# Low parts of twenty-six weight tiles moved from VectorE to GpSimd, in a windowed attention with two feed forwards

## The reference, cut to what matters

```python
# attention: q, k, v are (2, 8, 768, 64); each query sees 8 global keys and the last 96 keys, with a bias by distance
scores = scale * q @ k.T - slope * dist
a = exp(scores - max) / (sum + 1e-9)
x = (a @ v) as (1536 tokens, 512)
# first feed forward, w_in (512, 2048), w_out (2048, 512)
h = x @ w_in
g = (a0 + a1*h + a2*h**2 + a3*h**3) / (1 + |b0|*|h| + |b1|*h**2 + 1e-6)
x = g @ w_out
# second feed forward, w2_in (512, 1024), w2_out (1024, 512)
h = x @ w2_in
solu = h * softmax(h)
out = (layer norm of solu, times g_ln) @ w2_out
```

## Time and profile before

| what | value |
|---|---|
| median of 3 runs | 491.23 us (490.56 to 491.66) |
| the profiled execution | 491.82 us, of which the span is 489.9 us |
| PE busy | 480.8 us (98%) |
| DVE busy | 380.6 us (78%) |
| ACT busy | 262.9 us (54%) |
| GpSimd busy | 63.0 us (13%), all but 4.2 us of it before 94 us |
| chain that ended last | PE 86%, DVE 11%, ACT 2% |
| low parts of w_in on DVE | 16 instructions, 12.2 us |
| low parts of w_out on DVE | 8 instructions, 9.8 us |

### The profile page before, as it was taken

The page is one execution under the profiler, slowest core; times in us unless marked ns, Lnnn a source line. Parts: engine busy times, 40 slices in busy tenths (PEclk is TensorE's granted clock), DMA queues, the critical chain, the costliest instruction groups (busy, mean ns, idle before and its releaser), DMA issues.

```text
span 489.9 us, 7177 instructions
## 1 busy us (share of the span) xinstructions
PE 480.8 (98%) x2560; PEld 390.8 (80%) x2560; DVE 380.6 (78%) x705; ACT 262.9 (54%) x474; POOL 63.0 (13%) x133
## 2 busy tenths in 40 slices
PE   7999999999999999999999999999999999999997
PEld 5777667888888887888888788888888888888885
DVE  5899996899999789888878999999785554554450
ACT  4999895655454556544545655444444333433341
POOL 4767765200000000000000000000000000000000
PEclk9999999999999999999999999999999999999999
DMA  8699969600000000000032336332012222222201
GB/s 289 212 400 416 406 233 373 223 34 0 1 0 1 1 0 1 0 1 0 1 87 86 113 102 193 88 110 84 0 44 64 66 65 64 64 64 64 73 34 43
DMA packets 26959, 50.22 MB, mean 103 GB/s; under 512 B 2224, under 2 KB 16560, under 8 KB 25392
## 3 DMA queue, kind: packets, MB, share of 16 engines
q1 hardware_dynamic: 23760, 37.23, 21.9%
q0 software_dynamic: 2880, 12.58, 7.6%
q10 hardware_dynamic: 288, 0.01, 0.0%
HBM read 40.38 MB, written 3.15 MB: 89 GB/s over the span
## 4 chain that ended last, share of the span: by engine, by line
PE 86%; DVE 11%; ACT 2%; issue 1%; POOL 0%; POOLq 0%; DVEq 0%
PE ps L1102 9%; PE ps L1104 9%; PE ps L1103 9%; PE ps L1032 8%; PE ps L1033 8%; PE ps L1034 8%; PE ps L1167 4%; PE ps L1165 4%; PE ps L1122 4%; PE ps L1166 4%; PE ps L1121 4%; PE ps L1120 4%; DVE negs L653 3%; PE ps L1148 2%; DVE bank_a_lo L690 2%; PE ps L963 2%
## 5 line engine op out<-in xcount | busy, mean ns | idle before, releaser
L1102 PE MATMUL ps<-gate_hi,bank_b_hi 128*128 128x512 f32 x192 | 74.8, 390 | 0.5 <-DVE tok_lo L852 0.5
L1032 PE MATMUL ps<-tok_hi,bank_a_hi 128*128 128x512 f32 x192 | 75.1, 391 | 0.0
L1033 PE MATMUL ps<-tok_lo,bank_a_hi 128*128 128x512 f32 x192 | 74.7, 389 | 0.0
L1034 PE MATMUL ps<-tok_hi,bank_a_lo 128*128 128x512 f32 x192 | 74.7, 389 | 0.0
L1103 PE MATMUL ps<-gate_lo,bank_b_hi 128*128 128x512 f32 x192 | 74.7, 389 | 0.0
L1104 PE MATMUL ps<-gate_hi,bank_b_lo 128*128 128x512 f32 x192 | 74.7, 389 | 0.0
L494 ACT ACTIVATE quad<-ps 128x1024 f32<-128x1024 f32 x24 | 24.7, 1029 | 69.9 <-DVE rest L794 67.0
L412 POOL TENSOR_SCALAR probs<-probs,small 128x256 f32<-128x256 f32 (+1 forms) x96 | 48.6, 519 | 24.7 <-DVE small L663 24.0
L452 ACT ACTIVATE probs<-negs,small 128x256 f32<-128x256 f32 (+1 forms) x96 | 46.1, 485 | 6.0 <-DVE small L653 5.7
L776 DVE SCALAR_TENSOR_TENSOR quad<-quad,small,absh 128x1024 f32<-128x1024 f32 x24 | 30.8, 1283 | 21.5 <-ACT absh L497 21.4
L497 ACT ACTIVATE absh<-ps,small 128x1024 f32<-128x1024 f32 x24 | 26.8, 1116 | 33.8 <-PE ps L1104 33.8
(11 more groups left out here) (94 smaller groups left out, 948.3 us busy)
## 6 DMA issues: line engine op xcount, KB each, us to landing
v_sb<-in_v_win SPq DMA_DIRECT2D x8, 704.0 KB, 7.6
bank_a_raw<-in_w_in SPq DMA_DIRECT2D x4, 1024.0 KB, 11.2
bank_a_hi<-in_w_in POOLq DMA_DIRECT2D x4, 1024.0 KB, 9.9
bank_b_raw<-in_w_out SPq DMA_DIRECT2D x4, 1024.0 KB, 9.8
bank_b_hi<-in_w_out POOLq DMA_DIRECT2D x8, 512.0 KB, 5.6
q_sb<-in_q_t SPq DMA_DIRECT2D x16, 192.0 KB, 5.9
k_sb<-in_k_win SPq DMA_DIRECT2D x8, 384.0 KB, 7.2
stage_hi<-tok_hi SPq DMA_DIRECT2D x12, 256.0 KB, 2.7
```

The costliest lines, as they stand in the source:

```text
L1032: pe.matmul(banks(bank, 1), bank_a_hi[:, f, ws], x_hi, start=(k == 0), stop=False)
L1033: pe.matmul(banks(bank, 1), bank_a_hi[:, f, ws], x_lo, start=False, stop=False)
L1034: mm = pe.matmul(banks(bank, 1), bank_a_lo[:, f, ws], x_hi, start=False, stop=(k == KT - 1))
L1102: pe.matmul(banks(4 + k, 1), bank_b_hi[:, f, ws], g_hi, start=first, stop=False)
```

## The change: what it does

Of the 16 subtractions for w_in, DVE keeps the first six (`EARLY_IN`), now at blocks 34, 36, ... 44. The other ten and all eight for w_out go to GpSimd, behind its last transfer for w_out, in the order in which PE needs them: two tiles of w_out, then two of w_in. A new semaphore, `in_lo_late`, tells PE of the ten. SP loads w_in one step (six blocks) later, and GpSimd issues the high parts at blocks 14, 21, 28 and 35.

```diff
-    SPLIT_FROM, CAST_FROM, CAST_EVERY = 16, 10, 6
+    EARLY_IN, SPLIT_FROM, CAST_FROM, CAST_EVERY = 6, 34, 14, 7
...
-                if 1 <= k <= 4:
-                    load_w_in(k - 1)
+                if 2 <= k <= 5:
+                    load_w_in(k - 2)
...
         for j in range(EARLY_OUT, FT // 2):
             cast_w_out(j)
+
+        def split_in_low(f):
+            pool.wait_ge(in_loaded[f // 4], 16)
+            pool.wait_ge(in_hi_loaded[f // 4], 16)
+            pool.tensor_tensor(bank_a_lo[:, f, :], bank_a_raw[:, f, :], bank_a_hi[:, f, :].bitcast(F32),
+                               ALU.subtract).then_inc(in_lo_late, 1)
+
+        def split_out_low(j):
+            tiles = slice(2 * j, 2 * j + 2)
+            pool.wait_ge(outw_loaded[j // 2], 16)
+            pool.wait_ge(outw_hi_loaded[j], 16)
+            pool.tensor_tensor(bank_b_lo[:, tiles, :], bank_b_raw[:, tiles, :], bank_b_hi[:, tiles, :].bitcast(F32),
+                               ALU.subtract).then_inc(outw_lo_ready, 1)
+
+        for j in range(FT // 2):
+            split_out_low(j)
+            for f in (EARLY_IN + 2 * j, EARLY_IN + 2 * j + 1):
+                if f < FT:
+                    split_in_low(f)
...
             f, part = divmod(n - SPLIT_FROM, 2)
-            if part == 0 and 0 <= f < FT:
+            if part == 0 and 0 <= f < EARLY_IN:
                 split_in_low(f)
...
             dve.wait_ge(act_const, 1)
-            split_out_low(0)
             gate_poly(0)
...
             gate_rest(g)
-            if c == 0 and j + 1 < GROUPS:
-                split_out_low(j + 1)
-            elif c == CHUNKS - 1:
+            if c == CHUNKS - 1:
...
             if c == 0:
-                pe.wait_ge(in_lo_ready, f + 1)
+                if f < EARLY_IN:
+                    pe.wait_ge(in_lo_ready, f + 1)
+                else:
+                    pe.wait_ge(in_lo_late, f - EARLY_IN + 1)
```

More of the change, by code:

```diff
@@ L206, in attention_feed_forwards @@
     w2_hi_loaded = [sem(f"w2_hi_loaded{i}") for i in range(FT // 2)]
-    in_lo_ready, outw_lo_ready, w2_lo_ready = sem("in_lo_ready"), sem("outw_lo_ready"), sem("w2_lo_ready")
+    in_lo_ready, in_lo_late, outw_lo_ready, w2_lo_ready = (sem("in_lo_ready"), sem("in_lo_late"),
+                                                           sem("outw_lo_ready"), sem("w2_lo_ready"))
     hidden_ready, act_in_ready, quad_ready, poly_ready = sem("hidden_ready"), sem("act_in_ready"), sem("quad_ready"), sem("poly_ready")
@@ L805, in low_parts @@
                               ALU.subtract).then_inc(done, 1)
-        def split_out_low(j):
-            dve.wait_ge(outw_loaded[j // 2], 16)
-            dve.wait_ge(outw_hi_loaded[j], 16)
-            low_parts(bank_b_hi, bank_b_lo, bank_b_raw, j, outw_lo_ready)
         for h in range(2):
@@ L838, in _ @@
             full_attention()
-            for f in range(FT):
+            for f in range(EARLY_IN):
                 split_in_low(f)
```

## The result

The changed kernel takes 521.68 us (median of 4 runs, 521.32 to 522.16) against 491.35 us for the kernel before (4 runs, 490.56 to 491.66): 1.062 times as long, 95% interval 1.0602 to 1.0639. The forecast was slower, 501.0 us, in a range of 488 to 508. The direction was right, and the size was missed by 20.7 us.

What follows compares the result with a forecast made beforehand. PE, busy 98% of the span, was taken as the bound, losing time only where DVE or GpSimd delay it. Attention's -2.5 and the first chunk's +12.3 gave +9.8: 501.6 us profiled, 501.0 median, range 488 to 508.

Steps and rivals of the forecast that it cites:

- So they take turns by whole instructions, the one that waits comes next: First chunk: DVE's two-input gate instructions and GpSimd's subtractions alternate one by one; estimated cost +12.3 us.
- 3.7, 5.4 and 3.7: First chunk: PE's three main predicted waits in us, for gate_lo of groups 0, 1 and 2.
- the turns' changes given back: First chunk: each switch between DVE and GpSimd recovers 0.13 us, lowering the summed PE waits from 13.4 to 11.3 us.
- the ceiling of 2.44 and 1.36: First chunk: upper bound in us for GpSimd subtractions of 1024 and 512 elements.
- the prediction's walk: First chunk: instruction-by-instruction schedule of DVE, GpSimd and PE; +4.9 us at GpSimd's floor, +18.6 at its ceiling.
- the sum: Whole kernel: -2.5 us from attention and +12.3 from the first chunk make +9.8.
- rival 3: After the first chunk's stalls PE's clock falls to 1.2 GHz, adding 8 us, for 509 us; chance 6%.
- Attention, -2.5 us: Attention: with nine subtractions before block 34 gone from DVE, PE waits less; -2.5 us, between -1.6 and -3.6.
- The later loads I cost at nothing: Attention: loading w_in six blocks later costs nothing; if the last v came late, under 1 us.
- GpSimd's durations: First chunk: two-tensor subtractions on GpSimd take 1.98 us for 1024 elements and 1.12 for 512.
- Rival 1: First chunk: GpSimd's reads don't hold up DVE's gate, leaving only attention's gain; 488.7 us (487.6 to 489.6); chance 22%.
- Rival 2: First chunk: DVE gets the next turn more often and down(0) waits 1.4 us; 490 to 492 us; chance 8%.

## Why the prediction was wrong, and where it was right

**The step that failed** is "So they take turns by whole instructions, the one that waits comes next". It was read from a pair of L412 in attention, and there it held. But that pair stands behind a wait of GpSimd (0.22 us), and the new row stands right behind five DMA issues. One PE wait of 30.2 us took the place of three. Where GpSimd stops once between issues and row, the step holds, and PE waits three times: 3.33, 4.18 and 1.85 us, 9.4 together; with the stop behind the first subtraction 5.69, 2.00 and 3.43, together 11.1 (3.7, 5.4 and 3.7 were worked out, and with the turns' changes given back 11.3 in all).

That these runs stand at 502.8 and 504.0 us, near the 501.0 of the forecast, is in part luck. The subtractions took 2.36 and 1.28 us, close to the ceiling of 2.44 and 1.36 for which the prediction's walk gives +18.6. Against that, a change of turns gave back more than 0.13 us: a gate instruction and a subtraction of 512 took 2.15 us together (L816 to L819, 94.31 to 96.46) where their own times of 1.26 and 1.28 add up to 2.54. And the clock, which the sum left out, cost some 3 us, as shown under rival 3.

Could the trace of before have shown it? Four rows of L412 there stand right behind a DMA issue, and one of them meets a two-input instruction of DVE:

```profile
42.15 0.58 POOL L399 DMA_DIRECT2D bank_a_hi<-in_w_in  x1
42.77 2.21 POOL L412 TENSOR_SCALAR probs<-probs,small 128x256 f32<-128x256 f32 x4
...
44.06 0.68 DVE L690 TENSOR_TENSOR bank_a_lo<-bank_a_raw,bank_a_hi 128x512 fp32r<-128x512 f32 x1
```

L690 got in at once, and GpSimd's last L412 took 909 ns. These are one-tensor pieces of 365 to 504 ns, shorter than any that held DVE in the experiments, so this row looks like turns and warns of nothing. The trace of before has no row of long GpSimd instructions behind an issue. The prediction treated one collision of two short instructions as a rule for eighteen long ones, and gave no chance to DVE's getting no turn.

**Attention, -2.5 us**: -2.8 was measured, of which 0.3 was there by 14 us, and -2.5 in the run without GpSimd's subtractions. The term was right. "The later loads I cost at nothing": v is late by 0.63 us, since the load took 11.3 us where 8.3 were assumed. With the loads as before PE waited 0.91 us for v, 1.47 for k and 0.67 for a copy, but in an execution of 491.53 us, the slowest of seven. The medians differ by 0.9 us in favour of the later ones, and the intervals overlap: the term was small and, if anything, of the other sign.

**GpSimd's durations**, 1.98 and 1.12 us: 2.36 and 1.28 in the row, within the ceiling. The Trainium skill's 4497 ns for 2048 elements ("GPSIMD Engine Reference", section "Performance versus the Vector engine"), halved to 2.25, was closer than my estimate.

**Rival 1**, no hold-up, 488.7 us: not what happened, but its number is that of the kernels whose row doesn't hold DVE, 489.17 with memsets and 489.51 with short pieces. Its "24 us at 1.98 and 1.12" is a slip: 8 x 1.98 + 10 x 1.12 is 27.0, and nothing else in the prediction rests on it. **Rival 2**, DVE favoured: not with whole subtractions, but with pieces of 128x128 it is what happened. The gate ran at 1.3 to 1.5 us an instruction and down(0) waited 2.86 us for GpSimd, where the rival had 1.4.

**Rival 3**, the clock: the prediction had it fall after stalls of 3.7 us, at 8 us in all and a chance of 6%. In the changed kernel it came after one stall of 30 us and cost 2.9. It counts in the runs with turns too. With the stop ahead of the row the granted clock was 0.82 from 96 to 102 us and 0.72 from 116 to 122. Behind PE's first two waits 17 steps from matmul to matmul took 0.37 to 0.50 us where 0.227 is usual, 3.4 us lost. The span grows by 11.1 us there; -2.6 from attention (up(0) at 76.40), 9.4 of waits and 3.4 of clock make 10.2. With the stop behind the first subtraction, and with one behind each, such steps cost 3.1 and 4.1 us. So stalls of 3.3 to 5.7 us did lower the clock; the rival priced a real term about twice too high, and the sum, which had nothing for it, was wrong to leave it out.

**What stays open.** Why a DMA issue leaves GpSimd in this state, and where the limit in duration lies below which instructions let DVE in nonetheless (396 and 442 ns did, 630 and 717 did not, 521 to 572 did once after nine), isn't settled. The stop, the issue inside the row and the one pause were each run once. That the stop has to be one in which GpSimd really waits is inferred: the row's waits for loads that had landed long before cleared nothing.

## What to carry to other kernels

Work that is moved to GpSimd beside two-input DVE work is priced by what it does to DVE, and one collision in a trace tells only of its own circumstances: look whether GpSimd had just waited or just issued a transfer. A wait on the engine's own completion between its DMA issues and a row of SBUF reads turns a hold into turns, which here still cost 12 us (502.80 against 490.98). To lose nothing, let each instruction go by a semaphore of DVE's so that it runs beside PSUM readers (488.64). When an instruction has a mean of twice its known length, look for a single long one before explaining an average.

## What the runs showed of the hardware that was not expected

- A row of GpSimd instructions that read SBUF, behind a DMA issue without a stop, kept one DVE instruction with two inputs in SBUF waiting for 31.97 us (18 instructions) and 36.74 us (52); DVE's PSUM readers ran in 1.21 to 1.28 us beside GpSimd's subtractions (L803 and L805 in the run with the issue inside the row, the latter behind the issue).
- A stop of 0.08 us turned this into turns by whole instructions, for the rest of the row; one DMA issue in the row brought the hold back.
- Cutting 18 subtractions into 52 made the hold longer (526.25 against 521.68 us); cutting them into 104 removed it (495.61), and then GpSimd was the one that waited.
- After PE waits of 3.3 to 5.7 us in the runs with turns the granted clock was down, and matmuls were 0.43 us apart instead of 0.227 for about 3 us and more.
